# The copy of the first head's rows of q is issued ahead of the stores of x, in the attention's SyncE program

## What is computed

```python
q_rot, k_rot = (rotate(q), rotate(k))
scores = scale * np.matmul(q_rot, k_rot.transpose(0, 1, 3, 2))
scores = scores - np.max(scores, axis=-1, keepdims=True)
attn = np.exp(scores)
attn = attn / (np.sum(attn, axis=-1, keepdims=True) + 1e-09)
attn_out = np.matmul(attn, v)
# x = attn_out with the heads side by side: (4, 576, 512)
h = np.maximum(x.transpose(0, 2, 1) @ w_tok1, 0.0) @ w_tok2
u = x + h.transpose(0, 2, 1)
return u + np.maximum(u @ w_ch1, 0.0) @ w_ch2
```

## Time and profile before

| | us |
|---|---|
| median of 3 runs (639.83 to 644.56) | 640.11 |
| the profiled execution's own time | 641.5 |
| its span | 639.5 |
| PE busy | 601.7 (94%) |
| DVE busy | 445.1 (70%) |
| ACT busy | 387.2 (61%) |
| POOL busy | 274.1 (43%) |

### The profile page before, as it was taken

How to read it: one execution, slowest core, us unless ns; L and a number is a source line. 1 busy time by engine, 2 the same in 40 slices (tenths; PEclk the granted TensorE clock), 3 DMA queues, 4 the chain that set the end, 5 groups by cost and what they waited for, 6 DMA issues and landing times.

```text
span 639.5 us, 19511 instructions
## 1 busy us (share of the span) xinstructions
PE 601.7 (94%) x7796; PEld 553.3 (87%) x7796; DVE 445.1 (70%) x844; ACT 387.2 (61%) x725; POOL 274.1 (43%) x240
## 2 busy tenths in 40 slices
PE   2999999989989889899999999999999999999997
PEld 1788878778777778788999999999999999999996
DVE  5577777757767767774655985569935499553895
ACT  3566666756656657764473665776556765567753
POOL 4666577766556655326500002860017800068200
PEclk9999999989999999999999999999999999999999
DMA  5234534444444553216001332000320003100002
GB/s 136 72 103 134 140 98 130 116 127 126 117 130 107 162 147 105 63 43 201 1 1 49 151 84 74 1 2 2 84 74 0 0 0 82 48 28 1 1 2 75
DMA packets 49870, 48.18 MB, mean 75 GB/s; under 512 B 12800, under 2 KB 42048, under 8 KB 49792
## 3 DMA queue, kind: packets, MB, share of 16 engines
q1 hardware_dynamic: 49488, 47.00, 25.4%
q10 hardware_dynamic: 304, 0.07, 0.0%
HBM read 30.24 MB, written 9.44 MB: 62 GB/s over the span
## 4 chain that ended last, share of the span: by engine, by line
PE 80%; DMA 7%; DVE 4%; SPq 4%; issue 2%; ACT 1%; DVEq 0%
PE rest L632 9%; PE slot L592 9%; PE slot L1115 8%; PE slot L1117 8%; PE slot L1116 8%; DMA moved_q<-turned_q 7%; PE rest L1115 6%; PE rest L1117 6%; PE rest L1116 6%; PE rest L531 6%; SPq L432 3%; PE slot L588 3%; PE slot L1147 2%; PE rest L1147 1%; DVE x_pair L832 1%
## 5 line engine op out<-in xcount | busy, mean ns | idle before, releaser
L800 DVE TENSOR_REDUCE neg_max<-slot 128x1 f32<-128x576 f32 x144 | 106.5, 755 | 41.4 <-PE slot L592 34.5
L1106 POOL TENSOR_TENSOR w_ch_part<-w_ch_sums,w_ch_part 128x512 fp32r<-128x512 f32 x21 | 31.0, 1475 | 180.3 <-ACT w_ch_part L1357 180.3
L723 ACT ACTIVATE pt<-rest 128x320 f32<-128x320 f32 x144 | 62.5, 434 | 71.5 <-PE rest L531 70.5
L592 PE MATMUL slot<-turned_k,turned_q 64*128 64x288 f32 x256 | 86.3, 442 | 20.6 <-DMA moved_q<-turned_q 18.3
L1421 ACT ACTIVATE pieces<-h 128x288 fp32r<-128x288 f32 x168 | 73.8, 444 | 49.8 <-PE slot L1117 24.9
L632 PE MATMUL rest<-v,pt 128*64 128x65 f32 x2880 | 103.5, 226 | 0.0
L632 PEld LDWEIGHTS rest<-v,pt 128*64 128x64 f32 x2880 | 92.2, 139 | 10.6 <-ACT pt L723 5.8
L809 DVE COPY pt<-rest 128x320 f32<-128x320 f32 x144 | 70.0, 486 | 35.0 <-PE rest L531 34.5
L592 PE MATMUL slot<-moved_k,moved_q 64*128 64x288 f32 x256 | 86.8, 444 | 0.0
L1512 DVE TENSOR_TENSOR pieces<-h,pieces 128x288 fp32r<-128x288 f32 x168 | 74.1, 451 | 9.4 <-ACT pieces L1421 8.8
L714 ACT ACTIVATE prob_a<-slot,neg_max 128x576 f32<-128x576 f32 x80 | 59.2, 740 | 17.5 <-DVE neg_max L800 14.4
(11 more groups left out here) (236 smaller groups left out, 1793.4 us busy)
## 6 DMA issues: line engine op xcount, KB each, us to landing
moved_q<-turned_q SPq DMA_DIRECT2D x31, 160.0 KB, 2.5
raw_qk<-in_q_dram SPq DMA_DIRECT2D x16, 256.0 KB, 2.6
raw_v<-in_v_dram SPq DMA_DIRECT2D x16, 256.0 KB, 2.7
x_scratch<-x_pair SPq DMA_DIRECT2D x16, 256.0 KB, 2.0
stage_or_x<-x_scratch SPq DMA_DIRECT2D x16, 256.0 KB, 4.1
raw_qk<-in_k_dram SPq DMA_DIRECT2D x15, 256.0 KB, 2.9
w_ch_whole<-in_moe_w_ch_dram SPq DMA_DIRECT2D x8, 384.0 KB, 3.4
w_ch_A_whole<-in_moe_w_ch_dram SPq DMA_DIRECT2D x4, 768.0 KB, 8.0
```

Source lines behind the costliest of these rows:

```text
L592: mm = pe.matmul(s[:, r, 0:HALF], x[:, cols], w, start=True, stop=True, skip_group_check=True)
L723: act.activation(pt_of(p, i)[:, :, top], rest[:, 0, 0:NG * D].rearrange("p (j n) -> p j n", j=NG), ACT.Copy).then_inc(up_done, 1)
L800: dve.tensor_reduce(neg_max[p % 2][:, i:i + 1], score_slot(p, i)[:, :, 0:HALF], AX.XY, ALU.max, negate=True).then_inc(maxed, 1)
```

## The change

In each pair, SP issues the copy of head A's rows of q directly after that of its k, and the three stores of x_pair after it. The waits stand with their DMAs: SP now waits for turned_q first (`t_done["q"]`) and for the normalised x (`x_done`) behind it. Nothing else is changed.

```diff
@@ -451,8 +451,8 @@
             if not no(p + 1):
                 sp.wait_ge(scores, p * TILES + G + 1)
             move("k", 0, p + 1)
+            move("q", 0, p + 1)
             store(p - 1)
-            move("q", 0, p + 1)
             load_next("k", p + 3)
             sp.wait_ge(scores, (p + 1) * TILES)
             move("k", 1, p + 1)
```

## The result

Four runs of the changed kernel have a median of 622.83 us (621.01 to 624.19), beside 642.34 for four runs of the kernel before (639.83 to 645.25). The ratio is 0.969, with an interval from 0.963 to 0.975: faster by 3%. Two more series of the same changed kernel gave 0.973 (0.967 to 0.979) and 0.973 (0.971 to 0.976). The forecast was 624.3 us, range 620.5 to 633.

A forecast was written before the change was run, and what follows sets the result against it. PE bounds the kernel, with 18.3 us of waits for the moved_q copy. Gains 3.4 + 3.5 + 0.3 + 7.1 + 1.5 = 15.8 us take 641.5 to 625.7, 1.4 less for the median: 624.3 us, range 620.5 to 633.

The forecast's parts named there:

- PE stands still for the copy, the copy stands behind the stores' issues: Starts of pairs 2 to 15: PE waits 14 times for moved_q, 18.3 us, the copy issued 0.90 us after turned_q.
- Kind A: Five of PE's 14 waits for moved_q, 0.67 to 0.71 us each, vanish with 0.19 us to spare; gain 3.4 us.
- Kind B: Three waits for moved_q (1.11, 1.62, 1.60 us), where an instruction packet holds SP's store issue; gain 3.5 us.
- Kind C near: Three waits for moved_q (0.93, 0.95, 1.58 us), mostly staying because a packet still catches the earlier copy; gain 0.3 us.
- the packets come at places of PE's program that should stay where they are relative to turned_q: Instruction packets on queue q8, about every 6 us, were expected at fixed places relative to turned_q; no size of its own.
- Kind C far: Three waits for moved_q (2.63, 2.28, 2.18 us); earlier copies slip past packets 2.2 to 2.3 us after issue; gain 7.1 us.
- The rival by which the packet would still catch it: Packets 2.2 to 2.3 us after issue still hold the copies; 7.1 and 1.5 us not gained, 632.9 us; chance 0.16.
- The clock: Half granted clock from 134.20 to 137.50, behind PE's 2.63 us wait, was expected to stay away; gain 1.5 us.
- The stores: Issued behind the copy, x_pair's last store lands 3.4 to 5.4 us after turned_q, before DVE's L832 at 5.55: covered.
- the rival of late stores: Stores landing over 5.55 us after turned_q stall DVE at L832, then ACT and PE; 1 us late costs 14; chance 0.04.

## Why the prediction was right, and where it was not

- **PE stands still for the copy, the copy stands behind the stores' issues**: right. 0.90 us between turned_q and the copy became 0.03, the waits went from 18.3 to 2.4 us (2.8 and 2.1 in the repeats). The large store ahead costs nothing, the small ones ahead cost what their issues take, and the load of k ahead costs its issue too: it is SP's time and not the data in the queues.
- **Kind A, 3.4 us** (pairs 1, 4, 7, 10, 13): right, none of the five waits is left in any profile of the changed kernel. The margin was mis-sized. I took PE as ready 2.89 us after turned_q, from the listed wait. In pair 0 it starts 2.73 after (31.34 - 28.61); in pair 1 of the changed kernel, with the landing of 2.7 us, it starts 2.86 after (45.55 - 42.69), without being listed as waiting. So the spare 0.19 us was not there. Each removed wait was worth up to 0.2 us more than its row says (16.42 a pair against 15.54, for a listed wait of 0.68), and the large store behind takes 0.17 of it back.
- **Kind B, 3.5 us** (pairs 8, 11, 14): the sum was near, 3.3 in this profile (4.3 us of waits became 1.0), a step wrong, and that the errors cancel is luck. I expected the copy itself to be held when it is issued 0.3 us into a packet. In the two pairs with that in the profile after (2 and 11), it was not: its issue took the usual time and it landed in 2.7 and 2.5 us. Of the three pairs two have no wait, 0.8 us more than I had given them; pair 8 has a new one of 1.04, by a packet that started 1.2 us after its copy's issue, so its gain of 1.1 did not come. (The packet's row, of 155.2 to 155.3: 85.4% x 1.6 = 1.37 us; the copy was issued at 154.07 and PE went on at 157.98.) A hold of SP hit what was issued behind other DMAs, as in the row at 106.71 below, where the small stores took 1.77 us instead of 1.1 and nobody waited for them.

```profile
q8 instruction: 1, 0.02, 85.4%
```

```profile
105.55 0.48 SPq L422 DMA_DIRECT2D moved_q<-turned_q  x1
106.08 0.58 SPq L429 DMA_DIRECT2D x_scratch<-x_pair  x1
106.71 1.77 SPq L432 DMA_DIRECT2D x_scratch<-x_pair  x2
```

- **Kind C near, 0.3 us** (pairs 2, 3, 5): mis-sized, 2.3 in this profile (3.5 us of waits became 1.15), since it was reckoned pair by pair with packets standing still. The step that failed is "the packets come at places of PE's program that should stay where they are relative to turned_q". The pattern over three pairs stays; but in the three profiles of the changed kernel the packet of pair 5 came at + 1.5, + 2.7 and - 0.3, that of pair 2 at - 0.3, + 1.2 and + 1.2. Two to four of 14 copies are caught or late in each, for 2.1 to 2.8 us. I had left 4 us of waits, the greater part in these three pairs.
- **Kind C far, 7.1 us** (pairs 6, 9, 12): the mechanism is right: the packet starts near the copy's end or behind it instead of amid it, and at most 0.3 us of waits is left in the three pairs, in every profile of the changed kernel and in the one with these pairs alone. The size is that of one execution: in the repeat of the kernel before, the same pairs had 4.9 us to give, not 7.1. The rival by which the packet would still catch it is true at the edge: one full catch at 2.13 us, and 0.2 to 0.5 us at 2.5 to 2.7. The Trainium skill, "DMA: Bandwidth & Descriptors", section "Queues, rings and completion order", has the semaphore increment land only after every earlier write of its engine; the catch at 2.13, just before a free copy's landing, would agree with that. But seven packets at 2.26 to 2.37, as short before landings of 2.33 to 2.39, held nothing, and the copies with a packet at 2.5 to 2.7 landed after 2.8 to 3.2, which is 0.4 to 0.7 us before that packet's own end. So the runs here do not show this rule at work.
- **The clock, 1.5 us**: right that it goes with the long waits, though a wait's length alone does not decide: 2.28 and 2.18 us in the profile before brought no dip, 1.96 in its repeat did. It is a matter of each execution: in three profiles of the stores-first order (before, its repeat, and the change in three pairs) there were one, two and no dips inside the attention, and none in three profiles of the changed kernel. With the copy behind k's load, where eight waits were 2.2 us or longer, there were eight. The profile before, with one dip, has a mean granted clock of 0.997, its repeat, with two, 0.994. The 18 runs of the kernel before beside that repeat have 0.987 to 1.000 with a median of 0.995, the 13 runs of the changed kernel 0.998 to 1.000. So a run of before had about one or two dips (an estimate from these clocks), and the term was worth 1.5 to 3 us.
- **The stores**: right that they are covered. The last one landed 3.7 to 5.4 us after turned_q (to 5.6 in a repeat), and DVE never waits for them in the changed kernel; 1.3 us later it does, in four pairs. The price in the rival of late stores, a microsecond of PE for each of DVE, was too high: 3.3 us of DVE's wait cost nothing measurable, and 24.4 cost 20.
- **What the sum did not have**: the start, 1.46 us of the difference between the two profiles, which is no gain of the change. Without it the profiled execution gained 18.1 us, 2.3 more than my 15.8: 1.6 from waits I had thought would stay, 0.7 from the unlisted part of each wait. Over the runs the two later series put the changed kernel at 624.0 and 624.1 us, beside the forecast's 624.3. That closeness is in part luck: the gains over the kernel before in the same series are 19.5, 17.1 and 16.8 us, 1 to 4 more than the 15.8, and the 640.11 that the forecast started from is 0.7 to 2.2 us lower than the medians of before in these series.

## What to carry to other kernels

On an in-order queue that issues DMAs, an issue of 0.3 to 0.6 us is work like any other: what a waiting engine needs next goes first, and what nobody waits for goes behind it, as far as its buffer's next writer allows. A wait of one transfer need not be moved past all that stands ahead of it; whatever was ready before it can stay. Count the pairs (here 12 of 14) in which the moved instruction really exists, and take the time an engine is ready from a pair without the wait, not from the listed wait.

## What the runs showed of the hardware

A fetch of instructions, one packet of 0.02 MB that occupies one DMA engine for 0.9 to 1.8 us (once 2.4), about every 6 us in this attention, holds up a copy of 160 KB inside SBUF if it starts 0.4 to 1.6 us after the copy's issue: in all 37 cases the copy landed 1.2 to 1.5 us after the packet's end, instead of 2.3 to 2.7 us after its issue. "Mostly hidden", as the Trainium skill says in "Runtime: NRT & Kernel Launch", section "Instruction fetch mechanics", is true here of the program that is fetched (PE was busy all 15.54 us from 26.45 to 41.99, with three fetches begun in them), and not of a transfer on the path: it cost 0.7 to 1.3 us of PE's time each of the six times it caught one fully in the three profiles of the changed kernel.

A store of 256 KB issued right behind a copy inside SBUF of 160 KB makes the copy land 0.3 us later (2.39 to 2.69 in pair 1), while the same store 0.7 us ahead of it does not.
